# Turning K ahead of the exponentials' turns, and the normalised x one step later, in a fused attention and MLP kernel

## The chip, the cores and the metric

One core of one Trainium2 chip runs the whole program. The metric is the device time of one execution in microseconds. All stages are one launch; nothing is computed on the host but the layout of the arrays.

## The reference

`q`, `k`, `v` are (4 batches, 12 heads, 448 positions, 64). What matters here is the first part and what it hands on:

```python
def rmsnorm(x, g):
    rms = np.sqrt(np.mean(x * x, axis=-1, keepdims=True) + 1e-06)
    return x / rms * g
q_n, k_n = (rmsnorm(q, g_q), rmsnorm(k, g_k))
scores = scale * np.matmul(q_n, k_n.transpose(0, 1, 3, 2))
scores = scores - np.max(scores, axis=-1, keepdims=True)
attn = np.exp(scores)
attn = attn / (np.sum(attn, axis=-1, keepdims=True) + 1e-09)
out = np.matmul(attn, v)                    # then x = out as (4, 448, 768)
# layer 1
xn = (x - mu) / np.sqrt(var + 1e-06) * g_ln
x = x + np.maximum(xn @ w_ch1, 0.0) @ w_ch2
# layer 2
u = x + (x.transpose(0, 2, 1) @ U @ V).transpose(0, 2, 1)
out = u + np.maximum(u @ w_ch1, 0.0) @ w_ch2
```

## The kernel before

The work of each engine is written out by hand in one list of entries, `seq`, which every engine's program walks in the same order. Its first part is attention: entries ("step", n), n from 0 to 101. The 48 heads make 24 pairs, `t`; the 448 query positions make four tiles, `i`, of 112. So n = 4t + i, and I call the four steps of one t a period, and a step by its i. From step 96 on the products of the first MLP are mixed in, and from step 102 on there are only products. Engines run freely against each other and meet by semaphores alone, so an engine works through its own list in order, and stands still at the first entry whose semaphore has not come.

In step n TensorE does, in this order: `score(n)` (L696, six products of high and low parts of q and k), `value(n-2)` (L717, e turned times v), `turn_e(n-1, h)` for both heads (L704, four transposes of a 112 x 448 tile of exponentials each). In the step with i = 2 come `turn_k(t+1)` (L684, four transposes of the normalised K of the next pair) and `turn_values(t-1)` (L726) behind it; in the steps with i = 3 `turn_x("x", ...)` (L738, the pair's attention output turned for the residual), and, in 18 of the steps, `turn_x("n", ...)` (the same line, the layer-normalised x turned for the MLP). All turns except K's go into two PSUM banks, `sc_ps`, used in turn; a bank is free again when ScalarE or VectorE has copied it out. With e(n-1, 0) and e(n-1, 1) before it, any third turn of a step goes into the bank of e(n-1, 0), which ScalarE copies in `copy_e` (L869). The other one is VectorE's (L1045).

ScalarE's step: `keep_x` (L880) or `keep_norm` (L897) for a turn of the step before, `make_high` (L917, in steps 65 to 92 with i under 3: inputs of the MLP), `copy_e(n-1)` (L869), `exponential(n)` (L857, one for each head, with an accumulator read behind each), at i = 2 `k_high(t+1)` (L848), at i = 1 `keep_values(t-1)` (L865) and `q_high(t+1)` (L843), and `normalise` (L888, half of the layer norm of a tile) one step ahead of the tile's turn. GpSimd does the other half (L630), the roots (L560, L565, L588), K's scaling `norm_k` (L570), `sums` (L577) and Q's low part (L581). VectorE does maxima (L1034, L1040), copies of e, K's low part `k_low` (L1026), sums of squares (L1018), `natural` (L1057) and statistics.

The table `XN_AT` says in which step each normalised tile is turned: tiles of batch 0 at steps 32, 36, ... 52 (i = 0), of batch 1 at 56, 57, 60, 64, 68, 72, of batch 2 at 80, 84, ... 96 and 100. `XN_AT`'s steps also set the time of the two halves of `normalise`, of `keep_norm`, and of the DMA that stores the tile.

Of the kernel before, what the change touches and what calls it, by code (L numbers as in the profile page):

```python
# [29 lines left out]
def mixer_kernel(nc, qkv, q_t, g_qk2, g_ln, u_lr, v_lr, w1, w2, out_t):  # L30
# [142 lines left out]
    with ExitStack() as ctx:  # L173
# [124 lines left out]


        XN_AT = {}  # L300
        for b, (first, order, ats) in enumerate(((32, (0, 1, 2, 3, 4, 5), (0, 4, 8, 12, 16, 20)),
                                                 (56, (0, 3, 1, 2, 4, 5), (0, 1, 4, 8, 12, 16)),
                                                 (80, (0, 1, 2, 3, 4, 5), (0, 4, 8, 12, 16, 20)))):
            for c, at in zip(order, ats):
                XN_AT[first + at] = PB * b + c
        xn_no = {t: k for k, t in enumerate(list(XN_AT.values()) + list(range(NP_ - PB, NP_)))}

        def xn_pair(n):
            return XN_AT.get(n)
# [93 lines left out]
        with nc.Block() as block:  # L403
# [135 lines left out]
            def _(pool):  # L539
# [99 lines left out]
                for what, n in seq:  # L639
                    if what == "step":  # L640
                        t, i = divmod(n, NI)
                        if i == 0:
                            for s, c, k in sum_made_at.get((what, n), ()):
                                make_sum(s, c, k)
                            if xn_pair(n + 1) is not None:
                                normalise(xn_pair(n + 1))
                        if i == 0 and t + 1 < NP_:
                            root_k(t + 1)
                            norm_k(t + 1)
                            root_q(t + 1)  # L650
                        if i == 1 and 1 <= t <= NP_:
                            sums(t - 1)
                        if i == 2 and t + 1 < NP_:
                            q_low(t + 1)
                        if i == 3 and t + 2 < NP_:
                            squares(t + 2)
                        if i == 0 and t >= 1 and (t - 1) % PB == 0 and t > 1:
                            root_var((t - 1) // PB - 1)
                        if i == 3 and xn_pair(n + 1) is not None:
                            normalise(xn_pair(n + 1))  # L660
                        if i != 0:
                            for s, c, k in sum_made_at.get((what, n), ()):
                                make_sum(s, c, k)
                        continue
                    for r, k in sums_at.get(n, ()):
                        weight_sum(r, k)
                    if what == "prod":
                        for s, c, k in sum_made_at.get((what, n), ()):
                            make_sum(s, c, k)

            @block.tensor
            def _(pe):
# [6 lines left out]
                def turn_k(t):  # L679
                    pe.wait_ge(kn_done, t + 1)  # L680
                    wait(pe, av_done, t - 1)
                    to = k_turned(t)
                    for i in range(NI):
                        last = nc.tensor.transpose(to[:, i * TP:(i + 1) * TP], kn[:, i], ident[:TP, :TP])  # L684
                    last.then_inc(kt_done, 1)
# [126 lines left out]
                for what, n in seq:  # L812
                    if what == "step":
                        if n < N:
                            score(n)
                        if 1 <= n <= 2:
                            warm((7, 6)[n - 1])
                        if 0 <= n - 2 < N:
                            value(n - 2)
                        for h in range(2):  # L820
                            if 0 <= n - 1 < N:
                                turn_e(n - 1, h)
                        if n % NI == 2 and n // NI + 1 < NP_:
                            turn_k(n // NI + 1)
                        if n % NI == 2 and 1 <= n // NI <= NP_:
                            turn_values(n // NI - 1)
                        if xt_pair(n) is not None:
                            turn_x("x", xt_pair(n))
                        if xn_pair(n) is not None:
                            turn_x("n", xn_pair(n))  # L830
                    if what == "prod":
                        if ln3_pair(n - 2) is not None:
                            turn_x("n", ln3_pair(n - 2))
                        if (at := mix_of(n)):
                            mixing(*at)
                        product(n)

            @block.scalar
            def _(act):
# [119 lines left out]
                for what, n in seq:  # L959
                    if what == "step":  # L960
# [6 lines left out]
                            make_high(s, c, k)  # L967
                        if 0 <= n - 1 < N:
                            copy_e(n - 1)
                        if n < N:  # L970
                            exponential(n)
                        if i == 2 and t + 1 < NP_:
                            k_high(t + 1)
                        if i == 1 and 1 <= t <= NP_:
                            keep_values(t - 1)
                        if i == 1 and t + 1 < NP_:
                            q_high(t + 1)
                        if xn_pair(n + 1) is not None:
                            normalise(xn_pair(n + 1))
# [283 lines left out]
```

## Time and profile before

| | |
|---|---|
| median of 3 runs | 1703.59 us (1701.42 to 1703.87) |
| profiled execution | 1705.68 us, its span 1703.7 us |
| PE busy over the span | 1666.4 us (98%), weight loads 1486.2 us (87%) |
| DVE, ACT, POOL busy | 1097.4, 701.5, 484.2 us |
| the chain that ended last | PE 80%, of it the products L770 41% and L760 35% |
| attention, until the first product of the MLP | 349.66 us of the span |

In the views PE is TensorE, PEld its weight loads, DVE VectorE, ACT ScalarE, POOL GpSimd and SP the queue that issues the DMAs. Times are in us from the span's start. In a timeline a row says when the first instruction of a group started and how long the group lasted; brackets say how long the engine had been idle before it, and what released it. On ACT and PE a row's duration overlaps with the next row's start, since instructions are pipelined: the time that one takes in the queue is read from start to start.

### The profile page before, as it was taken

To read this page: it belongs to the slowest core of one execution; us is meant where nothing else is said; L and a number is where in the kernel's file an instruction comes from. 1 tells how busy PE (TensorE), PEld (TensorE's weight loads), DVE (VectorE), ACT (ScalarE), POOL (GpSimd) and SP (SyncE) were. 2 spreads that over 40 slices of the span, in tenths; PEclk is the share of its full clock that TensorE was granted. 3 is DMA by queue.
4 is the path that set the end of the run, shared out by engine and by line. 5 is a ranking of instruction groups with operands and counts; after the bars stand their busy time and mean duration, and the time that the engine had idled before them with its cause. 6 is when DMAs were issued, how large, how long until landed. Compare 5 with 4: busy or idle time off the path is not lost.

```text
span 1703.7 us, 27419 instructions
## 1 busy us (share of the span) xinstructions
PE 1666.4 (98%) x10040; PEld 1486.2 (87%) x10040; DVE 1097.4 (64%) x2072; ACT 701.5 (41%) x1648; POOL 484.2 (28%) x434
## 2 busy tenths in 40 slices
PE   9999988899999999999999999999999999999999
PEld 7767666689999999999999999999999999999998
DVE  6878788866555559665555496656555975555654
ACT  5777888752233224332232243223322432223321
POOL 5667778711111114211021132110111321111110
PEclk9999999999999999999999999999999999999999
DMA  4223334221112114422221145122211451111112
GB/s 122 76 73 88 93 104 132 65 91 65 67 67 75 42 59 158 169 78 77 78 78 61 55 164 183 62 75 81 93 49 67 164 171 44 62 62 56 56 56 84
DMA packets 54867, 149.29 MB, mean 88 GB/s; under 512 B 6000, under 2 KB 36848, under 8 KB 54736
## 3 DMA queue, kind: packets, MB, share of 16 engines
q1 hardware_dynamic: 54736, 147.55, 26.5%
q8 instruction: 82, 1.34, 0.3%
q14 instruction: 49, 0.40, 0.1%
HBM read 122.75 MB, written 24.77 MB: 87 GB/s over the span
## 4 chain that ended last, share of the span: by engine, by line
PE 80%; DVE 1%; ACT 1%; issue 1%; POOL 1%; DVEq 0%; ACTq 0%; POOLq 0%
PE mm_ps L770 41%; PE mm_ps L760 35%; PE sc_ps L782 1%; PE sc_ps L792 1%; PE mm_ps L717 0%; PE mm_ps L696 0%; PE sc_ps L738 0%; ACT e_nat L857 0%; PE sc_ps L800 0%; PE sc_ps L704 0%; DVE mm_ps L1034 0%; DVE h_lo L1100 0%; ACT e_t L869 0%; DVE qk_ss L1018 0%; POOL make L601 0%
## 5 line engine op out<-in xcount | busy, mean ns | idle before, releaser
L770 PE MATMUL mm_ps<-h_hi,w_hi 128*128 128x448 f32 x1152 | 423.1, 367 | 0.0
L770 PE MATMUL mm_ps<-h_hi,w_lo 128*128 128x448 f32 x1152 | 421.0, 365 | 0.0
L770 PE MATMUL mm_ps<-h_lo,w_hi 128*128 128x448 f32 x1152 | 420.9, 365 | 0.0
L1133 DVE TENSOR_TENSOR acc<-mm_ps,acc 128x448 f32<-128x448 f32 x288 | 166.2, 618 | 362.0 <-PE mm_ps L770 362.0
L760 PE MATMUL mm_ps<-in_hi,w_hi 128*128 128x448 f32 x1008 | 371.3, 368 | 0.0
L760 PE MATMUL mm_ps<-in_hi,w_lo 128*128 128x448 f32 x1008 | 368.3, 365 | 0.0
L760 PE MATMUL mm_ps<-in_lo,w_hi 128*128 128x448 f32 x1008 | 368.2, 365 | 0.0
L907 ACT ACTIVATE w_hi<-w_raw 128x256 fp32r<-128x256 f32 (+1 forms) x480 | 204.5, 452 | 188.7 <-PE mm_ps L770 168.1
L770 PEld LDWEIGHTS mm_ps<-h_hi,w_lo 128*128 128x128 f32 x1152 | 216.4, 188 | 17.6
L770 PEld LDWEIGHTS mm_ps<-h_lo,w_hi 128*128 128x128 f32 x1152 | 216.5, 188 | 17.0
L770 PEld LDWEIGHTS mm_ps<-h_hi,w_hi 128*128 128x128 f32 x1152 | 216.4, 188 | 17.0
L1087 DVE TENSOR_TENSOR w_lo<-w_raw,w_hi 128x256 fp32r<-128x256 f32 (+1 forms) x480 | 229.4, 491 | 0.3
L760 PEld LDWEIGHTS mm_ps<-in_hi,w_lo 128*128 128x128 f32 x1008 | 189.3, 188 | 15.3
L941 ACT ACTIVATE h_hi<-ht 128x448 fp32r<-128x448 f32 x144 | 83.4, 579 | 289.0 <-DVE ht L1118 155.7
L760 PEld LDWEIGHTS mm_ps<-in_lo,w_hi 128*128 128x128 f32 x1008 | 189.5, 188 | 14.6
L760 PEld LDWEIGHTS mm_ps<-in_hi,w_hi 128*128 128x128 f32 x1008 | 189.3, 188 | 14.6
L623 POOL TENSOR_TENSOR w_s<-w_raw,w_s 128x384 f32<-128x384 f32 x48 | 50.2, 1046 | 510.5 <-DVE w_lo L1087 510.5
L623 POOL TENSOR_TENSOR w_s<-w_raw 128x384 f32<-128x384 f32 x48 | 56.4, 1176 | 477.0 <-DMA w_raw<-in_w 407.7
L857 ACT ACTIVATE e_nat<-mm_ps,nbias,rs 112x448 f32<-112x448 f32 x192 | 137.5, 726 | 13.8 <-DVE nbias L1040 13.8
L1100 DVE SCALAR_TENSOR_TENSOR h_lo<-ht,h_hi 128x448 fp32r<-128x448 f32 x144 | 109.1, 758 | 32.2 <-ACT h_hi L941 32.1
L907 ACT ACTIVATE w_hi<-w_s 128x384 fp32r<-128x384 f32 x144 | 73.9, 517 | 116.2 <-POOL w_s L623 68.8
L1034 DVE TENSOR_REDUCE mm_ps<-mm_ps 112x2 f32<-112x896 f32 x96 | 104.8, 1092 | 9.1 <-PE mm_ps L696 9.0
(105 smaller groups left out, 1976.8 us busy)
## 6 DMA issues: line engine op xcount, KB each, us to landing
w_raw<-in_w SPq DMA_DIRECT2D x96, 768.0 KB, 4.3
qk<-in_qkv SPq DMA_DIRECT2D x23, 448.0 KB, 3.7
acc<-xres SPq DMA_DIRECT2D x6, 1344.0 KB, 9.8
qt_raw<-in_q_t SPq DMA_DIRECT2D x24, 224.0 KB, 2.6
v<-in_qkv SPq DMA_DIRECT2D x24, 224.0 KB, 2.7
xnrm<-st_n SPq DMA_DIRECT2D x24, 224.0 KB, 2.0
xres<-acc SPq DMA_DIRECT2D x24, 224.0 KB, 2.2
xa<-xres SPq DMA_DIRECT2D x24, 224.0 KB, 2.7
```

Of the source, the lines that this page charges most:

```text
L623: nc.gpsimd.tensor_tensor(out, in0, in1, op).then_inc(sum_done, 1)
L760: last = nc.tensor.matmul(bank(q), w[a][:, c * P:(c + 1) * P], x[:, k, c], start=k not in ONTO and c == 0 and p == 0, stop=c == HC - 1 and ...
L770: last = nc.tensor.matmul(bank(q, b), w[a][:, c * P:(c + 1) * P], x[:, half, 2 * c + b], start=half == 0 and c == 0 and p == 0, stop=half ...
L782: last = nc.tensor.matmul(sc_ps[1][:, :2 * P], u_st[:, i].rearrange("p n r -> p (n r)"), x[:], start=i == 0 and x is xs_hi, stop=i == NI - ...
L792: last = nc.tensor.transpose(sc_ps[0][:TP, e * P:(e + 1) * P], xa[:, e, i * TP:(i + 1) * TP], ident[:])
L857: nc.scalar.activation(e_nat[:, n % 3, h], mm_ps[:TP, 2 * (n % 2) + h, :S], ACT.Exp, bias=nbias[:, n % 2, h:h + 1], scale=rs[:, t % 2, 0, ...
L907: nc.scalar.activation(w_hi[:, q % RING, :width(q)], weights(q), ACT.Copy).then_inc(whi_done, 1)
L941: nc.scalar.activation(h_hi[:, g % 2, h], src, ACT.Relu).then_inc(hhi_done, 1)
L1034: nc.vector.reduce_max(nmax(n), mm_ps[:TP, 2 * (n % 2):2 * (n % 2) + 2, :S], axis=AX, negate=True).then_inc(max_done, 1)
L1087: nc.vector.tensor_tensor(w_lo[:, q % RING, :w], weights(q), w_hi[:, q % RING, :w].bitcast(F32), ALU.subtract).then_inc(wlo_done, 1)
L1100: nc.vector.scalar_tensor_tensor(h_lo[:, g % 2, h], src, 0.0, h_hi[:, g % 2, h].bitcast(F32), ALU.max, ALU.subtract).then_inc(hlo_done, 1)
L1133: nc.vector.tensor_tensor(acc[:, b, d], bank(q, b), acc[:, b, d], ALU.add).then_inc(ev_done, 1)
```

## The change

K's transposes stand ahead of e's on TensorE, K's high part ahead of the exponentials on ScalarE, Q's high part one step sooner, and the tiles in `XN_AT` are turned one step later (one of the last batch stays at step 100). GpSimd's half of `normalise` stays in the same step as before (it is called two steps ahead now), ScalarE's moves with the table.

```diff
-        for b, (first, order, ats) in enumerate(((32, (0, 1, 2, 3, 4, 5), (0, 4, 8, 12, 16, 20)),
-                                                 (56, (0, 3, 1, 2, 4, 5), (0, 1, 4, 8, 12, 16)),
-                                                 (80, (0, 1, 2, 3, 4, 5), (0, 4, 8, 12, 16, 20)))):
+        for b, (first, order, ats) in enumerate(((33, (0, 1, 2, 3, 4, 5), (0, 4, 8, 12, 16, 20)),
+                                                 (57, (0, 3, 1, 2, 4, 5), (0, 1, 4, 8, 12, 16)),
+                                                 (81, (0, 1, 2, 3, 4, 5), (0, 4, 8, 12, 16, 19)))):
...
-                            if xn_pair(n + 1) is not None:
-                                normalise(xn_pair(n + 1))
+                            if xn_pair(n + 2) is not None:
+                                normalise(xn_pair(n + 2))
...
-                        if i == 3 and xn_pair(n + 1) is not None:
-                            normalise(xn_pair(n + 1))
+                        if i == 3:
+                            for u in (xn_pair(n + 1), xn_pair(n + 2)):
+                                if u is not None:
+                                    normalise(u)
...
+                        if n % NI == 2 and n // NI + 1 < NP_:
+                            turn_k(n // NI + 1)
                         for h in range(2):
                             if 0 <= n - 1 < N:
                                 turn_e(n - 1, h)
-                        if n % NI == 2 and n // NI + 1 < NP_:
-                            turn_k(n // NI + 1)
...
+                        if i == 2 and t + 1 < NP_:
+                            k_high(t + 1)
                         if n < N:
                             exponential(n)
-                        if i == 2 and t + 1 < NP_:
-                            k_high(t + 1)
                         if i == 1 and 1 <= t <= NP_:
                             keep_values(t - 1)
-                        if i == 1 and t + 1 < NP_:
+                        if i == 0 and t + 1 < NP_:
                             q_high(t + 1)
```

On TensorE, in a step with i = 2 (here step 10, from its value product on: L717 value, L704 e's turns, L684 K's, L726 the values' turn, then the next score), before:

```order
L717 MATMUL mm_ps<-e_t,v 64x112 x8
L704 MATMUL sc_ps<-ident,e_nat 112x112 x8
L684 MATMUL mm_ps<-ident,qk_sq 128x112 x4
L726 MATMUL sc_ps<-ident,av 112x128 x4
L696 MATMUL mm_ps<-k_hi,q_hi 112x448 x2
```

and with the change, where lines stand two further down in the file:

```order
L719 MATMUL mm_ps<-e_t,v 64x112 x8
L686 MATMUL mm_ps<-ident,qk_sq 128x112 x4
L706 MATMUL sc_ps<-ident,e_nat 112x112 x8
L728 MATMUL sc_ps<-ident,av 112x128 x4
L698 MATMUL mm_ps<-k_hi,q_hi 112x448 x2
```

K's four transposes moved from between e's and the values' turns to ahead of e's, so that the values' turn follows e's directly.

On ScalarE, in steps 35 to 38, that is from the copy of e in step 35 (i = 3) to the one of step 38 (i = 2), before (L869 copy of e, L857 exponentials, L888 normalise, L880 keep x, L897 keep the normalised x, L865 keep values, L843 Q's high part, L848 K's):

```order
L869 ACTIVATE e_t<-sc_ps 112x448
L857 ACTIVATE e_nat,esum<-mm_ps,nbias,rs 112x448 x2
L888 ACTIVATE x_nat<-x_nat,shift,rstd 112x128 x2
L880 ACTIVATE acc<-sc_ps 128x448
L869 ACTIVATE e_t<-sc_ps 112x448
L857 ACTIVATE e_nat,esum<-mm_ps,nbias,rs 112x448 x2
L897 ACTIVATE st_n<-sc_ps,g_col 128x448
L869 ACTIVATE e_t<-sc_ps 112x448
L857 ACTIVATE e_nat,esum<-mm_ps,nbias,rs 112x448 x2
L865 ACTIVATE av<-mm_ps 128x448
L843 ACTIVATE q_hi<-qt_raw 128x448
L869 ACTIVATE e_t<-sc_ps 112x448
```

and with the change:

```order
L871 ACTIVATE e_t<-sc_ps 112x448
L859 ACTIVATE e_nat,esum<-mm_ps,nbias,rs 112x448 x2
L882 ACTIVATE acc<-sc_ps 128x448
L871 ACTIVATE e_t<-sc_ps 112x448
L859 ACTIVATE e_nat,esum<-mm_ps,nbias,rs 112x448 x2
L845 ACTIVATE q_hi<-qt_raw 128x448
L890 ACTIVATE x_nat<-x_nat,shift,rstd 112x128 x2
L871 ACTIVATE e_t<-sc_ps 112x448
L859 ACTIVATE e_nat,esum<-mm_ps,nbias,rs 112x448 x2
L867 ACTIVATE av<-mm_ps 128x448
L899 ACTIVATE st_n<-sc_ps,g_col 128x448
L871 ACTIVATE e_t<-sc_ps 112x448
```

Q's high part and both normalising instructions now stand between the exponentials of the step with i = 0 and the copy of e in the step with i = 1; the other steps have lost one or the other. The orders of GpSimd and VectorE are the same before and after; on SP only the stores of the normalised x stand one step later.

## Rows read from the trace of the kernel before

**Rows 1.** Windows: length, busy us of PE, PEld, DVE, ACT, POOL; granted clock; DMA.

```profile
62.15:75.14 12.99, 12.19 (x133) 9.16 (x132) 10.72 (x22) 9.69 (x26) 7.55 (x6) 1.00 0.25 72
143.53:156.94 13.41, 12.71 (x139) 9.51 (x138) 10.89 (x22) 10.86 (x29) 9.11 (x9) 1.00 0.29 87
302.14:316.16 14.02, 12.72 (x137) 9.53 (x137) 12.39 (x25) 12.29 (x32) 9.89 (x10) 1.00 0.22 67
...
0.00:349.66 349.66, 317.15 (x3293) 240.03 (x3293) 277.98 (x546) 265.95 (x652) 235.41 (x206) 0.99 0.31 92
349.66:1703.70 1354.04, 1349.26 (x6751) 1246.13 (x6749) 819.45 (x1527) 435.52 (x996) 248.78 (x228) 1.00 0.26 87
```

**Rows 2.** TensorE's waits in attention: waiter, releaser: us in total, times, longest.

```profile
PE sc_ps L738 <- ACT e_t L869: 10.1, 30, 0.3
PE mm_ps L717 <- DVE e_t L1045: 4.8, 11, 0.9
PE mm_ps L696 <- DVE k_lo L1026: 4.7, 6, 1.6
PE sc_ps L738 <- POOL x_nat L630: 4.4, 3, 2.2
PE sc_ps L726 <- ACT e_t L869: 4.3, 9, 0.5
...
PE sc_ps L704 <- ACT st_x L880: 0.8, 2, 0.6
```

**Rows 3.** Timeline of TensorE in step 18 (i = 2, a period without normalised x).

```profile
68.70 0.99 PE L717 MATMUL mm_ps<-e_t,v 112*64 112x112 f32 x16 [0.37 <-DVE e_t L1045]
69.62 0.98 PE L704 MATMUL sc_ps<-ident,e_nat 112*112 112x112 f32 x8
70.44 0.55 PE L684 MATMUL mm_ps<-ident,qk_sq 112*128 112x112 f32 x4
71.06 0.62 PE L726 MATMUL sc_ps<-ident,av 128*112 128x128 f32 x4
```

**Rows 4.** Timeline of GpSimd and ScalarE beside that step.

```profile
68.65 1.04 POOL L570 TENSOR_TENSOR qk_sq<-qk,rs 112x512 f32<-112x512 f32 x1
69.91 0.58 ACT L843 ACTIVATE q_hi<-qt_raw 128x448 fp32r<-128x448 f32 x1
70.37 0.55 ACT L869 ACTIVATE e_t<-sc_ps 112x448 f32<-112x448 f32 x1
```

**Rows 5.** Timeline of ScalarE, steps 39 and 40 (i = 3 and 0), with normalised x.

```profile
142.33 0.54 ACT L869 ACTIVATE e_t<-sc_ps 112x448 f32<-112x448 f32 x1 [1.10 <-PE sc_ps L704]
142.77 0.72 ACT L857 ACTIVATE e_nat<-mm_ps,nbias,rs 112x448 f32<-112x448 f32 x1
...
144.18 0.87 ACT L888 ACTIVATE x_nat<-x_nat,shift,rstd 112x128 f32<-112x128 f32 x2
144.95 0.54 ACT L880 ACTIVATE acc<-sc_ps 128x448 f32<-128x448 f32 x1
145.87 0.54 ACT L869 ACTIVATE e_t<-sc_ps 112x448 f32<-112x448 f32 x1 [0.39 <-PE sc_ps L704]
```

**Rows 6.** Timeline of TensorE in step 40: e's turns, then the normalised x's.

```profile
145.24 0.98 PE L704 MATMUL sc_ps<-ident,e_nat 112*112 112x112 f32 x8
146.56 0.57 PE L738 MATMUL sc_ps<-ident,x_nat 112*128 112x112 f32 x4 [0.34 <-ACT e_t L869]
```

**Rows 7.** Timeline of ScalarE and TensorE in step 86 (i = 2, with the MLP's inputs made).

```profile
310.91 0.58 ACT L917 ACTIVATE in_hi<-make 128x448 fp32r<-128x448 f32 x1
...
312.07 0.62 PE L726 MATMUL sc_ps<-ident,av 128*112 128x128 f32 x4 [0.54 <-ACT e_t L869]
```

**Rows 8.** Timeline of TensorE in steps 88 and 89: the longest wait, and what follows it.

```profile
321.02 0.86 PE L738 MATMUL sc_ps<-ident,x_nat 112*128 112x112 f32 x4 [2.17 <-POOL x_nat L630]
...
323.20 1.67 PE L717 MATMUL mm_ps<-e_t,v 112*64 112x112 f32 x16
```

**Rows 9.** Timeline of TensorE at step 32, the first of a period behind a late K.

```profile
115.52 0.46 PE L696 MATMUL mm_ps<-k_hi,q_hi 64*112 64x448 f32 x2 [0.93 <-DVE k_lo L1026]
```

## The prediction

> **What bounds the kernel now.** I first took the busy time of each engine by stage [rows 1]. From 349.66 us on TensorE is busy 1349.26 of 1354.04 us: nothing in the change touches that stage but its first steps, and whatever attention gains or loses shifts all of it. Before, TensorE is busy 317.15 of 349.66 us, so some 32 us of idleness are all that can be won. It is near to being the bound in every kind of period: 12.19 of 12.99 us in a plain one, 12.71 of 13.41 with a normalised x, 12.72 of 14.02 where the MLP's inputs are made too. ScalarE's share goes up from 9.69 to 10.86 and 12.29 us in the same three windows: in the last it has 1.7 us left in 14, so the place of a work in its queue matters more than its length. Then I read who TensorE waits for [rows 2]: the turns of x wait for ScalarE's copy of e 30 times, 0.34 us each, value for VectorE's copy 11 times, the values' turn for ScalarE's copy 9 times. Three waits for GpSimd make 4.4 us, six for K's low part 4.7. Last I read the timeline of a plain and of two fuller periods [rows 3 to 9].
>
> One relation carries the argument. A third turn of a step needs the bank that ScalarE empties: e's turns start at 145.24, the copy at 145.87 (0.63 later, when the first head is turned), the next turn at 146.56 (0.69 after the copy's start) [rows 5, 6]. So behind a turn of e, any third turn starts 1.32 us after e's start; e's eight transposes themselves take 0.82 (69.62 to 70.44) [rows 3].
>
> **K ahead of e's turns.** Nothing is added or removed, and K's high part isn't what the next score waits for: VectorE takes it up a step later. In a plain period K's transposes fill the time in which ScalarE copies: e's turn 69.62, K's 70.44, the values' 71.06 [rows 3], which is 0.69 after the copy's start at 70.37 [rows 4]. With K first, e's turn starts later by K's transposes: four instead of eight, so half of 0.82, 0.41 us. K is also ready only at 69.69 (68.65 and 1.04) [rows 4], against the slot at 69.62: some 0.1 more. That gives e's turn at 70.13, the copy at 70.76, the values' turn at 71.45: 0.4 us late. Bounds: 0.3, if GpSimd's end costs nothing and ScalarE, freed of Q's high part, copies with no delay; 0.5 with a later K. I take 0.4. Exponentials start later too, but they have over 1 us of slack: ScalarE idles 1.10 us ahead of the next copy [rows 5]. Steps 4 to 27 hold 6 such periods: **+2.4 us**. In the period that ends in step 31, VectorE gets its sums late from GpSimd and the next score waits 0.93 us for K's low part [rows 9]; the delay vanishes in that wait. I count the same for the other three periods that end in a large wait of this kind: 0.
>
> In periods with a normalised x but no MLP inputs, ScalarE was hardly late, so the same move costs K's 0.41 less a tenth by which the two copies of e had been late there: 0.3. Where inputs are made, ScalarE does them between Q's high part and the copy (310.91), and the values' turn waited up to 0.54 us [rows 2, 7]. Q's high part gone from there, and K first: I count 0.2 won.
>
> **Normalised x one step later, Q's high part sooner.** Take step 40 of before. ScalarE copies e at 145.87; 0.44 later the exponentials (as 142.33 to 142.77), which with their reads take 1.41 (142.77 to 144.18): it is free at 147.72. Q's high part costs 0.46 from start to start (69.91 to 70.37) and the two normalising instructions 0.77 (144.18 to 144.95) [rows 4, 5]. Before, the second stood at the end of step 39, where 0.39 us of idleness were still left behind keep x, the first a step later. Now both follow the exponentials: ScalarE is free at 148.95. Without x's turn, step 41's score starts at 145.24 + 0.82, say 146.1; e's turn comes 1.71 later (143.53, the window's start, to 145.24), with a little wait for VectorE at 147.9, and can be copied from 148.5 [rows 1, 5, 6]. The copy is 0.45 us late, and with it x's turn and all behind it. Together with K's 0.3: +0.75 for each of 4 periods (steps 36 to 51), **+3.0**. Bounds of this lateness: 0, if the high part of Q or the normalising slips into idle time, to 0.9. The period with two turns (57, 58) I put at +0.4, the one of 61 at +0.2, the last (no K, no Q) at +0.1.
>
> Where MLP inputs are made, one more instruction of some 0.48 from start to start (0.58 long) [rows 7] stands ahead of that copy: 0.93 late, less the 0.2 of K: +0.7. That holds in 4 periods (turns at 65, 73, 81, 85): **+2.8**. In the other two GpSimd was late, and a step's delay hides that. The three waits for it are 4.4 us, one of 2.17 and two of 1.1 [rows 2, 8]. For the turn at 69: 0.8 comes back of the 1.1, since 0.34 stays, against 0.7: 0. For the one at 81 I give nothing back, a choice: VectorE was late in that period as well, and puts the exponentials and the copy behind them back. For 89: x's turn waited 2.17 us, and TensorE then ran its value product in 1.67 us instead of 0.99 [rows 3, 8]; with e's turns (0.82) slowed in the same proportion that is 1.2 us for the fallen clock. 1.83 and 1.2 us come back, less 0.93, and K gives 0.2 but GpSimd's K is as much late: **-2.1**.
>
> Steps 32 to 35: the wait of 0.93 [rows 9] shrinks to some 0.5, since 0.4 of it now lies in step 30; if a fallen clock behind it (1.2 us) stays up instead, it is a gain of 0.5 beside the period's +0.7, and I put it at 0.1. At the end, normalise leaves the place ahead of keep x, where e's turn waited up to 0.6 us for the bank [rows 2]: **-0.6**. The stores of x move by a step of some 3.5 us and are needed 3 steps later: nothing.
>
> The Trainium skill (ScalarE: Activation LUTs, What ACT_TABLE_LOAD costs) says that back-to-back ACTIVATEs overlap by about 93 ns. The trace agrees: a copy lasts 0.54 us and holds the queue 0.44 [rows 5]. Costed by their durations, Q's part and the normalising would take 0.2 us more per period, and the sum would be some 2 us larger; I go by starts.
>
> **Sum.** 2.4 + 3.0 + 0.7 + 2.8 + 0 - 2.1 + 0.1 - 0.6 = +6.3 us. The profiled execution took 1705.68 us, so its like would take 1712.0; it was 2.1 us over the median of 1703.59, and against that I predict **1709.9 us**, 0.37% slower. What a measurement of this kernel can tell from no change is about 0.2%, 3.4 us.
>
> **Rivals.**
> *The queue on ScalarE isn't late (faster).* If the copy of e in steps with i = 1 comes on time, because the exponentials are through sooner than from 146.31 to 147.72 or the turn itself comes later, the terms for x shrink: 4 x 0.45 and 4 x 0.85 go, the two odd periods gain 0.9 each, the small ones 0.5: 7.5 us less, so -1.2. That decides from 0.4 us on in periods without MLP inputs and 0.9 us in those with them. A clock that then stays up behind the two longest waits for K's low part (up to 1.6 us [rows 2]), at 1.2 us each, brings it to -3.6: 1700.0, 0.2% faster. For it speaks that every one of the 4.4 us of waits for GpSimd goes; against it that ScalarE's queue is in order and its idleness ahead of the copy was 0.39 us in step 40 [rows 5], less than the 1.23 us that now come before.
> *The clock falls more often (slower still).* Behind the wait of 2.17 us the value product took 1.67 us [rows 8]. Full periods now have 0.34 + 0.93, near 1.3 us, of idleness in one place. Attention's granted clock is 0.99 as a whole [rows 1], so it fell seldom in before, with waits of 1.1 us among the rest; I don't count it. In four periods at 1.2 us each it is +4.8: 1714.7. The Trainium skill (TensorE: Matmul & The Clock Gate, Part 1) describes this: idleness halves the clock from 2.4 to 1.2 GHz and activity brings it back; the 1.67 us against 0.99 fit the lower level.
> *The waits only move (same).* If more of the K delay ends in a wait for K's low part or for VectorE's copy of e (0.37 in every plain period, 4.8 us in all [rows 2]), its 2.4 and the 1.2 in the next term vanish: +2.7, 1706.3. Against it: VectorE's copy comes ahead of K in the step, and its chain begins at the e turn of i = 0, which shifts along.
>
> **How the numbers follow.** Forecast, +4 to +9: 0.50. Clock: 0.13. Waits only move: 0.19. ScalarE not late: 0.18. The range reaches from the faster rival to beyond the clock's, since the bounds for ScalarE's lateness are wide: 1699.5 to 1716. Slower by over 0.2%: 0.63; within: 0.19; faster: 0.18.
>
> **What would show it.** Plain periods of 13.4 instead of 12.99 us, with the values' turn now waiting 0.3 to 0.4 us for ScalarE's copy in nearly every period, so that this wait grows from 4.3 to some 8 us. x's turns in steps with i = 1 waiting 0.7 to 1.3 us for the same copy: L738 on ACT up from 10.1 to some 17 us. The waits of L738 for GpSimd gone. If the first is wrong, K's transposes aren't 0.41; if the second is, ScalarE's queue was shorter than I counted. What follows 349.66 us should last as long as before, within 1 us.

## The result, and the profile after

| | before | changed |
|---|---|---|
| median of the runs side by side | 1702.63 us (5 runs, 1701.35 to 1703.87) | 1711.27 us (5 runs, 1710.62 to 1711.87) |
| ratio, 95% interval | | 1.0052, 1.0040 to 1.0063 |
| profiled execution, its span | 1705.68, 1703.7 us | 1710.62, 1708.7 us |
| attention, until the first product of the MLP | 349.66 us | 353.90 us |

The changed kernel is 8.6 us slower, 0.52%. I had said 1709.9 us, slower by 0.37%. The first windows are the whole of attention and all that follows, with the columns of [rows 1]; the other three are a plain period, one with a normalised x, and one that makes the MLP's inputs too.

```profile
0.00:353.90 353.90, 311.32 (x3289) 235.06 (x3289) 274.67 (x545) 265.87 (x649) 235.16 (x206) 1.00 0.31 91
353.90:1708.70 1354.80, 1349.99 (x6755) 1246.44 (x6753) 817.34 (x1527) 437.11 (x1000) 249.07 (x228) 1.00 0.26 86
...
63.93:77.71 13.78, 12.25 (x134) 9.18 (x133) 10.62 (x22) 9.79 (x26) 7.53 (x6) 1.00 0.23 68
147.66:161.78 14.12, 12.72 (x137) 9.53 (x136) 10.76 (x22) 10.92 (x29) 9.10 (x9) 1.00 0.28 83
309.17:323.76 14.59, 12.72 (x138) 9.54 (x137) 12.29 (x25) 12.36 (x32) 9.70 (x9) 1.00 0.20 64
```

Most of it lies in attention: 4.2 of the 5.0 us between the two profiles. The part behind it lasts 1354.80 us against 1354.04 [rows 1], and half of these 0.8 us is a border that moved: before, the normalised x of step 96 is turned at 349.31 us, just ahead of the first product; with the change, at step 97, it is turned at 356.84, behind it, and takes 0.37 us there. The busy times of each kind of period are those of before, and only the lengths have grown: 13.78 for 12.99, 14.12 for 13.41, 14.59 for 14.02. So work was not added; TensorE stands still for longer. Whom it waits for in attention, with the columns of [rows 2]:

```profile
PE sc_ps L740 <- ACT e_t L871: 21.3, 38, 1.2
PE sc_ps L728 <- ACT e_t L871: 7.7, 23, 0.3
PE mm_ps L719 <- DVE e_t L1047: 4.8, 10, 0.9
PE mm_ps L686 <- ACT av L867: 4.2, 9, 0.5
PE mm_ps L698 <- DVE k_lo L1028: 2.2, 4, 0.9
```

Against [rows 2], x's turns wait 21.3 us for ScalarE's copy of e instead of 10.1, the values' turn 7.7 instead of 4.3. The 4.4 us of waits for GpSimd's half of the normalising are gone, and K's low part costs 2.2 instead of 4.7. The fourth row has no counterpart in [rows 2]: **K's turn (L686) waits for ScalarE's copy of the kept values (L867)**, nine times, 0.47 us in the typical case. My prediction doesn't mention it. The step-18 timeline of TensorE, ScalarE and GpSimd, the place of [rows 3, 4], shows where it comes in:

```profile
70.44 1.04 POOL L570 TENSOR_TENSOR qk_sq<-qk,rs 112x512 f32<-112x512 f32 x1
...
70.49 0.99 PE L719 MATMUL mm_ps<-e_t,v 112*64 112x112 f32 x16 [0.37 <-DVE e_t L1047]
...
71.27 0.54 ACT L867 ACTIVATE av<-mm_ps 128x448 f32<-128x448 f32 x1
...
71.94 0.57 PE L686 MATMUL mm_ps<-ident,qk_sq 112*128 112x112 f32 x4 [0.47 <-ACT av L867]
72.36 0.93 PE L706 MATMUL sc_ps<-ident,e_nat 112*112 112x112 f32 x8
72.94 0.54 ACT L871 ACTIVATE e_t<-sc_ps 112x448 f32<-112x448 f32 x1 [1.14 <-PE sc_ps L706]
...
73.63 0.62 PE L728 MATMUL sc_ps<-ident,av 128*112 128x128 f32 x4 [0.34 <-ACT e_t L871]
```

GpSimd has K ready at 71.48 (70.44 and 1.04), and TensorE's value product is through at about the same time. But K is turned into the bank `mm_ps[:, 4 + t % 2]`, in which the values of the pair two before it (same remainder of t) were summed up, so `turn_k` has a second wait, on `av_done`: ScalarE must have copied those values out. That copy stands behind the exponentials of the step with i = 1 and ends at 71.81. K starts at 71.94. Before, the same copy stood here in step 18, beside [rows 4]:

```profile
69.48 0.54 ACT L865 ACTIVATE av<-mm_ps 128x448 f32<-128x448 f32 x1
```

It ended at 70.02, 0.4 us behind the slot at 69.62 into which K was to move. But e's eight transposes stood in that slot, K came at 70.44, and the wait was covered; K's position was what paid for it.

**Two profiles of the same kernel.** The difference of the two profiled spans is 5.0 us, that of the medians 8.6. So I profiled before once more (run e8_before_again below). Here are its windows, and TensorE at the place of [rows 8], from it:

```profile
0.00:345.78 345.78, 312.84 (x3292) 236.41 (x3293) 278.13 (x546) 266.17 (x652) 236.10 (x206) 1.00 0.32 93
345.78:1699.60 1353.82, 1349.02 (x6751) 1246.17 (x6749) 818.28 (x1527) 435.82 (x996) 249.45 (x228) 1.00 0.26 87
...
318.65 0.60 PE L738 MATMUL sc_ps<-ident,x_nat 112*128 112x112 f32 x4 [2.16 <-POOL x_nat L630]
...
319.97 0.99 PE L717 MATMUL mm_ps<-e_t,v 112*64 112x112 f32 x16
```

The wait of 2.16 us is there as in [rows 8], but the value product behind it lasts 0.99 us, not 1.67. The granted clock (the column ahead of the last two) behind this wait, TensorE alone, first in the first profile and then in the second:

```profile
322.00:324.00 2.00, 2.00 (x14) 0.50 0.29 108
318.65:322.00 3.35, 3.35 (x36) 1.00 0.21 72
```

Attention is 345.78 us long instead of 349.66, with a granted clock of 1.00 instead of 0.99. The first profile of before holds 3.9 us that this one doesn't: three places at which TensorE fell to the lower of its two levels (1.2 instead of 2.4 GHz) behind a wait, 1.2 us each, at steps 32, 64 and 88, and 0.3 us of smaller shifts. Against the second profile the change costs 1708.7 - 1699.6 = 9.1 us, near the 8.6 of the medians. In what follows I compare with the second one where a clock fall would blur a number.

By period (step n = 4t), the change against both profiles of before, in us, with what I had predicted:

| part | predicted | first profile | second profile |
|---|---|---|---|
| up to step 4 | 0 | -0.6 | -0.5 |
| six plain periods, t = 1 to 6 | +2.4 | +4.7 | +4.7 |
| t = 7, 13, 19 (end in a wait for K's low part) | 0 | -0.3 | -0.3 |
| t = 8 (begins with step 32) | +0.1 | -0.5 | +0.7 |
| four with a normalised x, t = 9 to 12 | +3.0 | +2.9 | +2.9 |
| t = 14 and 15 (steps 56 to 63) | +0.6 | +0.1 | +0.1 |
| t = 16, 18, 20, 21 (MLP inputs) | +2.8 | +1.4 | +2.5 |
| t = 17 (turn at 69) | 0 | -0.1 | -0.1 |
| t = 22 (turn at 89) | -2.1 | -2.2 | -0.6 |
| step 92 to the first product | -0.5 | -1.2 | -1.2 |
| behind it | 0 | +0.8 | +1.0 |
| sum | +6.3 | +5.0 | +9.1 |

Rounded as they are, the rows of the last column add up to 9.2. Some 0.4 us of the last two parts is the turn of x that changed sides.

### The profile page after: what moved, and what is told of

Its sections match the earlier page's. It is cut to its first block, busy times and chain, and to the rows that moved or that the text cites. A ratio compares the mean times of both kernels' runs of the same rounds, so it can differ in the third digit from the quotient of the medians.

```text
span 1708.7 us, 27419 instructions
## 1 busy us (share of the span) xinstructions
PE 1661.3 (97%) x10040; PEld 1481.5 (87%) x10040; DVE 1092.0 (64%) x2072; ACT 703.0 (41%) x1648; POOL 484.2 (28%) x434
## 4 chain that ended last, share of the span: by engine, by line
PE 80%; DVE 1%; ACT 1%; issue 0%; DVEq 0%; ACTq 0%
PE mm_ps L772 41%; PE mm_ps L762 35%; PE sc_ps L784 1%; PE mm_ps L719 1%; PE sc_ps L794 1%; PE mm_ps L698 1%; PE sc_ps L706 0%; PE sc_ps L740 0%; ACT e_t L871 0%; PE sc_ps L802 0%; ACT e_nat L859 0%; DVE mm_ps L1036 0%; DVE h_lo L1102 0%; PE sc_ps L728 0%; DVE x_nat L1015 0%
## 5 line engine op out<-in xcount | busy, mean ns | idle before, releaser
L762 PEld LDWEIGHTS mm_ps<-in_hi,w_hi 128*128 128x128 f32 x1008 | 189.4, 188 | 14.4
```

The source lines that it names most:

```text
L762: last = nc.tensor.matmul(bank(q), w[a][:, c * P:(c + 1) * P], x[:, k, c], start=k not in ONTO and c == 0 and p == 0, stop=c == HC - 1 and ...
```

## The experiments

Two theories stood. The first (A): K in front of e's turns costs nearly all of it, since its turn waits for the copy of the kept values, and with it 0.8 us in every plain period. The second, my prediction's: K costs 0.4 where nothing covers it, and the queue of ScalarE with the later normalised x and Q's high part costs the larger half, 3.5 of 6.3 us or more. In the texts on record and below, "before" is the kernel before, run beside each experiment, whose median was between 1702.4 and 1703.1 us.

### One part alone

**e1_k_alone**: before, with nothing but K moved, on TensorE and on ScalarE.

```diff
+                        if n % NI == 2 and n // NI + 1 < NP_:
+                            turn_k(n // NI + 1)
                         for h in range(2):
                             if 0 <= n - 1 < N:
                                 turn_e(n - 1, h)
-                        if n % NI == 2 and n // NI + 1 < NP_:
-                            turn_k(n // NI + 1)
...
+                        if i == 2 and t + 1 < NP_:
+                            k_high(t + 1)
                         if n < N:
                             exponential(n)
-                        if i == 2 and t + 1 < NP_:
-                            k_high(t + 1)
```

> Only K's part of the change: K's turn ahead of e's on TensorE, K's high part ahead of the exponentials. Theory A (the wait for the bank that the kept values leave is what K's turn pays for, and it is paid in every period whose i = 2 step isn't followed by a larger wait): in plain periods i = 2 steps last 4.9 instead of 4.14 us, and since Q's high part and the kept values still stand right ahead of the copy, the step grows by some 0.8 us in the periods with a normalised x too and by 0.4 where MLP inputs are made; TensorE waits for L865's copy in more than 15 steps; total +9 to +12 us against before, more than the whole change. Rival B (K first costs only its own transposes, 0.3 to 0.4 us a period, and the normalised x costs the rest): +4 to +6 us.

Measured: 1711.75 us, ratio 1.0053 (1.0039 to 1.0066), +9.3 us. K alone costs as much as the whole change. TensorE's waits in attention:

```profile
PE sc_ps L738 <- ACT e_t L869: 11.6, 35, 0.3
PE sc_ps L726 <- ACT e_t L869: 7.9, 23, 0.3
PE mm_ps L684 <- ACT av L865: 7.5, 17, 0.5
```

x's turns wait as before, the values' turn as in the changed kernel, and K's turn waits 17 times for the kept values, 7.5 us in all. Here the periods with a normalised x have the wait too: +0.78 in each of t = 9 to 12. K's high part ahead of the exponentials was not tried apart from K's turn; but TensorE's matmuls wait for no exponential, here or in the changed kernel, so nothing speaks for a cost of its own.

**e2_x_and_q**: the changed kernel with both moves of K taken back, so that the later normalised x and the sooner Q remain.

```diff
-                        if n % NI == 2 and n // NI + 1 < NP_:
-                            turn_k(n // NI + 1)
                         for h in range(2):
                             if 0 <= n - 1 < N:
                                 turn_e(n - 1, h)
+                        if n % NI == 2 and n // NI + 1 < NP_:
+                            turn_k(n // NI + 1)
...
-                        if i == 2 and t + 1 < NP_:
-                            k_high(t + 1)
                         if n < N:
                             exponential(n)
+                        if i == 2 and t + 1 < NP_:
+                            k_high(t + 1)
```

> The other part alone: normalised x one step later and Q's high part sooner, K where it was. Theory A: steps with i = 1 and a normalised x last 4.0 us (4.45 with MLP inputs) as in the changed kernel, steps with i = 2 shrink to 3.6 us, since nothing is ahead of the copy of e; the waits for GpSimd go. Total -3 to +1 us against before. Rival B (the later x is the costly part): +3 to +5 us.

Measured: 1702.41 us (11 runs; one of them took 5706.63 us and is not in the ratio), ratio 0.9998 (0.9989 to 1.0007). These two parts cost nothing together, where I had counted half of the loss. Yet the late copy that I had worked out is there, in this kernel as in the changed one:

```profile
PE sc_ps L740 <- ACT e_t L871: 19.4, 36, 1.3
...
PE mm_ps L698 <- DVE k_lo L1028: 3.9, 6, 1.2
...
PE sc_ps L706 <- DVE stats L1069: 1.3, 2, 0.7
```

Against the second profile of before, a plain period gains 0.12 (ScalarE's copy in the step with i = 2 is no longer late behind Q's high part), a period with a normalised x loses 0.31, the one with the wait of 2.16 us gains 1.5 and the end some 1.2.

The two parts are not additive by period. In t = 9 to 12 K alone costs 0.78 and x with Q 0.31, together 0.72. The steps with i = 1 are longer there in the changed kernel (3.99 us at step 37, before 2.62), so that ScalarE has copied the values before TensorE comes to K: one delay covers the other. In plain periods nothing covers it, and K on top of x and Q costs 0.90. Where MLP inputs are made (t = 18 and 21), K alone costs 0.3, x with Q 0.2, together 0.6.

### Taking the wait away

**e3_values_first**: the changed kernel, with the copy of the kept values in front of the exponentials in the step with i = 1.

```diff
-                        if n < N:
-                            exponential(n)
                         if i == 1 and 1 <= t <= NP_:
                             keep_values(t - 1)
+                        if n < N:
+                            exponential(n)
```

> The changed kernel with the values kept ahead of the exponentials of the step with i = 1 on ScalarE instead of behind them. Theory A: K's turn no longer waits 0.47 us for that copy in plain periods, but for GpSimd's K some 0.1 us; steps with i = 2 fall from 4.93 to 4.5 us in 7 to 9 periods, total 2.5 to 3.5 us below the changed kernel (about 1708). If K's turn was held by K's scaling on GpSimd anyway: no change, 1711.

Measured: 1708.17 us (1708.05 to 1708.51), 3.1 us below the changed kernel, ratio to before 1.0032 (1.0019 to 1.0045). The same step 18:

```profile
68.30 0.54 ACT L867 ACTIVATE av<-mm_ps 128x448 f32<-128x448 f32 x1
...
69.37 0.99 PE L719 MATMUL mm_ps<-e_t,v 112*64 112x112 f32 x16 [0.37 <-DVE e_t L1047]
...
70.42 0.60 PE L686 MATMUL mm_ps<-ident,qk_sq 112*128 112x112 f32 x4
70.86 0.93 PE L706 MATMUL sc_ps<-ident,e_nat 112*112 112x112 f32 x8
...
72.13 0.62 PE L728 MATMUL sc_ps<-ident,av 128*112 128x128 f32 x4 [0.34 <-ACT e_t L871]
```

The values are out at 68.84 and no longer hold K's turn. It starts 1.05 us behind the value product's start, where e's turn started 0.92 behind it before [rows 3]: GpSimd has K ready only at 70.36, the 0.1 that I had counted. A plain period now costs 0.40 over before, which is the term that I had predicted: without the bank's wait, my step was right. The other periods are as in the changed kernel.

**e7_k_values_first**: the same move in e1_k_alone.

```diff
+                        if i == 1 and 1 <= t <= NP_:
+                            keep_values(t - 1)
                         if n < N:
                             exponential(n)
-                        if i == 1 and 1 <= t <= NP_:
-                            keep_values(t - 1)
```

> K's part alone (as the run k alone), with the values kept ahead of the exponentials on ScalarE. Theory A: the 0.39 to 0.47 us of waiting for the kept values go in 17 steps, the rest of K first stays: i = 2 steps 4.5 us in plain periods, 4.1 with a normalised x; 5 to 7 us below K alone (1711.75): about 1706. Rival (the wait is really for GpSimd's K): 1709 to 1711.

Measured: 1707.80 us, 4.0 below e1_k_alone, ratio 1.0026 (1.0017 to 1.0034); each against the before beside it, +4.7 instead of +9.3. A plain period costs 0.40, one with a normalised x 0.35. My expectation was 5 to 7, a miss: K then meets its other feeder in the fuller periods (8 waits for GpSimd's scaling, 2.8 us). So 4.6 of the 9.3 us of K are the wait for the bank, 4.0 of them in the periods t = 1 to 6 and 9 to 12; of the 4.7 left, K's transposes in front of the copy make 3.8 in these ten periods (six by 0.40 and four by 0.35).

### The late copy on ScalarE

**e4_norm_early**: the changed kernel, with ScalarE's half of the normalising back in the step with i = 3 for the turns that come two steps later.

```diff
-                        if xn_pair(n + 1) is not None:
-                            normalise(xn_pair(n + 1))
+                        for u in (xn_pair(n + 1) if i == 3 else None, xn_pair(n + 2) if i in (3, 0) else None):
+                            if u is not None:
+                                normalise(u)
```

> The changed kernel with ScalarE's half of the normalising back in the step before (i = 3), as it was for a turn at i = 0, while x is still turned at i = 1. Theory A: the copy of e in i = 1 is on time again; x's turn waits 0.34 us instead of 0.71 and 1.17; the step lasts 3.62 instead of 3.99 and 4.45 us in 12 periods, total 6 to 8 us below the changed kernel (about 1704.5). If the normalising wasn't what made the copy late (Q's high part alone): under 2 us less.

Measured: 1709.11 us (1708.53 to 1710.09), ratio 1.0038 (1.0025 to 1.0050): only 2.2 us below the changed kernel, a miss. The changed kernel at step 41 first, with ScalarE's queue from the copy of step 40 on:

```profile
150.01 0.54 ACT L871 ACTIVATE e_t<-sc_ps 112x448 f32<-112x448 f32 x1 [1.16 <-PE sc_ps L706]
...
151.85 0.58 ACT L845 ACTIVATE q_hi<-qt_raw 128x448 fp32r<-128x448 f32 x1
152.08 0.98 PE L706 MATMUL sc_ps<-ident,e_nat 112*112 112x112 f32 x8
152.32 0.87 ACT L890 ACTIVATE x_nat<-x_nat,shift,rstd 112x128 f32<-112x128 f32 x2
...
153.09 0.53 ACT L871 ACTIVATE e_t<-sc_ps 112x448 f32<-112x448 f32 x1
...
153.77 0.57 PE L740 MATMUL sc_ps<-ident,x_nat 112*128 112x112 f32 x4 [0.71 <-ACT e_t L871]
```

and the same step in e4:

```profile
151.96 0.98 PE L706 MATMUL sc_ps<-ident,e_nat 112*112 112x112 f32 x8
...
152.59 0.54 ACT L871 ACTIVATE e_t<-sc_ps 112x448 f32<-112x448 f32 x1 [0.28 <-PE sc_ps L706]
153.27 0.57 PE L740 MATMUL sc_ps<-ident,x_nat 112*128 112x112 f32 x4 [0.34 <-ACT e_t L871]
```

The copy starts 0.63 after the turn instead of 1.01, x's turn waits 0.34 instead of 0.71, and all of L740's waits for ScalarE fall from 21.3 to 13.6 us: the edit did what it was made for. But periods of t = 9 to 12 win 0.34 each and three of the four with MLP inputs only some 0.3 (t = 16: 0.67) of the 0.76 to 0.90 that their step with i = 1 became shorter. With that step shorter, K's turn comes before the copy of the values again, and waits 0.46 (K on `av`: 6.4 us in all, from 4.2), value waits 0.86 for VectorE's copy of e in step 90, and at the end e's turn waits for the bank of x as it did before (0.8 us again). The cover of the last section, taken away, gives the price back.

**e6_all_fixed**: e4 and e3 together (its diff is those two).

> The whole change, with ScalarE's normalising in the step before and the values kept ahead of the exponentials. Theory A: what is left of K first is its own transposes and GpSimd's end, 0.3 to 0.4 us a period; K's turn waits no more for the kept values. i = 2 steps 4.5 us in plain periods, 4.0 with a normalised x. 4 to 5 us below the run with the normalising alone put back (1709.1): about 1704.5, and still 5 to 7 us above the same kernel with K where it was. Rival: K's wait for the kept values is replaced by a wait for K's scaling on GpSimd, over 1707.

Measured: 1707.35 us, ratio 1.0020 (1.0011 to 1.0029). I had expected about 1704.5, and the rival came (over 1707): the wait for the kept values is gone, that of x's turns is as in e4, and K's turn waits for its other feeder, GpSimd:

```profile
PE sc_ps L740 <- ACT e_t L871: 13.1, 36, 0.6
...
PE mm_ps L686 <- POOL qk_sq L570: 2.9, 8, 0.9
```

A plain period still costs 0.42 us, one with a normalised x 0.34, one with MLP inputs 0.2 to 0.3 over before (t = 18, 20 and 21; t = 16 nothing). That is what K's place costs when ScalarE holds up neither K nor x.

### Without K's move

**e5_no_k_norm_early**: e2 with the normalising as in e4.

> K where it was, normalised x turned one step later, Q's high part sooner, and ScalarE's half of the normalising in the step before (i = 3). Theory A (the two costs are separate: K's turn in front, and ScalarE's late copy of e in i = 1): both are absent, only the gains are left (waits for GpSimd gone, the values' turn not behind Q's high part): steps with i = 1 and a normalised x 3.6 us, with i = 2 3.6 us; 3 to 6 us below before, 1696.5 to 1699.5. If ScalarE's lateness only moves on to the i = 2 step: 1701 to 1703.

Measured: 1701.32 us, ratio 0.9985 (0.9976 to 0.9994), 1.8 us below before and 6.0 below e6, which differs from it in K's place and the values' copy. I had expected 1696.5 to 1699.5; it is the other case, that the lateness moves on to the step with i = 2. In the periods with MLP inputs the time went on to the next step: there e's second turn waits for the bank of the normalised x (L899, `keep_norm`), 3.0 us in six waits, since ScalarE's queue has exponentials and the values' copy in front of it. In step 86:

```profile
306.17 0.72 ACT L859 ACTIVATE e_nat<-mm_ps,nbias,rs 112x448 f32<-112x448 f32 x1 [0.78 <-DVE nbias L1043]
...
307.59 0.54 ACT L867 ACTIVATE av<-mm_ps 128x448 f32<-128x448 f32 x1
...
308.01 0.64 ACT L899 ACTIVATE st_n<-sc_ps,g_col 128x448 f32<-128x448 f32 x1
...
308.80 0.57 PE L706 MATMUL sc_ps<-ident,e_nat 112*112 112x112 f32 x4 [0.46 <-ACT st_n L899]
```

ScalarE idles 0.78 us for VectorE's maxima ahead of those exponentials, so the values' copy fits in there for nothing.

**e9_no_k_values_first**: e5 with the values' copy in front of the exponentials, the edit of e3.

> The kernel of the run no k, norm early (1701.3), with the values kept ahead of the exponentials in i = 1. There TensorE's second turn of e waits 0.37 to 0.46 us for ScalarE's copy of the normalised x (L899) in five i = 2 steps, 0.87 in one, while ScalarE idles 0.78 us ahead of the exponentials of the step before. If the copy of the values fits into that idleness (0.42 us from start to start), those waits go: 2 to 3 us less, about 1699. If VectorE's maxima end before it is through: 0 to 1 us less.

Measured: 1700.67 us (11 runs, 1698.85 to 1703.52), ratio 0.9986 (0.9977 to 0.9995). The waits for L899 fell from 3.0 us to 0.4. The median hardly moved, though (1701.32 before it, and the ratios to before are the same), where I had expected 2 to 3 us less. The runs with a granted clock of 1.0 took 1698.85 to 1699.24 us, against 1700.43 and 1700.49 in e5; before's own at 1.0 were some 0.4 us lower beside e9, so about 1 us was won there. The others took up to 1703.5, and waits for K's low part grew from 4.3 to 5.7 us. What was won in one wait is in part idleness of another.

**e10_root_later**: e9, with the roots of the layer norm (`root_var`, GpSimd, once for each batch) behind the sums of the next step.

```diff
                         if i == 1 and 1 <= t <= NP_:
                             sums(t - 1)
+                        if i == 1 and t >= 1 and (t - 1) % PB == 0 and t > 1:
+                            root_var((t - 1) // PB - 1)
...
-                        if i == 0 and t >= 1 and (t - 1) % PB == 0 and t > 1:
-                            root_var((t - 1) // PB - 1)
```

> The same, and GpSimd's root of the variance one step later, behind the sums of the exponentials (L577). At three places (steps 31, 55, 79) the sums now wait for it, and K's low part and the next score behind them, 0.65 to 0.94 us at the score and 0.6 to 0.75 at e's turn. If that root is what is late: some 1 us less at each, 2 to 4 us below the run before, about 1696. If VectorE would be as late without it: within 1 us of it.

Measured: 1696.90 us (1696.63 to 1697.74), ratio 0.9964 (0.9951 to 0.9976): 6.0 us faster than before, 14.4 faster than the changed kernel. GpSimd's sums in the period that ends in step 31 start at 109.40 instead of 110.96 us. TensorE in steps 31 and 32, first in e9:

```profile
112.72 0.57 PE L706 MATMUL sc_ps<-ident,e_nat 112*112 112x112 f32 x4 [0.58 <-DVE stats L1070]
113.12 0.55 PE L740 MATMUL sc_ps<-ident,x_nat 112*128 112x112 f32 x4
114.60 0.46 PE L698 MATMUL mm_ps<-k_hi,q_hi 64*112 64x448 f32 x2 [0.93 <-DVE k_lo L1029]
```

and in e10:

```profile
111.24 0.98 PE L706 MATMUL sc_ps<-ident,e_nat 112*112 112x112 f32 x8
112.56 0.58 PE L740 MATMUL sc_ps<-ident,x_nat 112*128 112x112 f32 x4 [0.34 <-ACT e_t L871]
113.06 0.46 PE L698 MATMUL mm_ps<-k_hi,q_hi 64*112 64x448 f32 x2
```

Both waits are gone, step 31 takes 3.54 us instead of 4.77, and steps 55 and 79 are 0.76 and 0.95 shorter.

### The same kernels again

**e8_before_again** and **e11_after_again** are before and the changed kernel, unchanged, for a second profile each.

> The kernel before, unchanged, for a second profile. The first one's execution took 2.1 us more than the median and had TensorE's clock fall behind three waits (steps 32, 64 and 88, about 1.2 us each). If the falls are a matter of the execution, this one shows another number of them and a span that differs by some 1.2 us for each; if they belong to the kernel, the same three and a span of 1703.7.

> The changed kernel once more, for a second profile: its waits ahead of steps 32, 64 and 89 are 0.3, 0.9 and 1.2 us instead of 0.9, 1.6 and 2.2. If TensorE's clock falls behind long waits alone, it stays up here too: span 1708.7 to 1710, granted clock 1.0. If not, falls of 1.2 us each appear at other places.

Measured: before 1701.56 us, its span 1699.6, as shown above; the changed kernel 1711.17, its span 1709.3, its periods within 0.02 us of the first profile's, the part behind attention 0.6 us longer. The 27 runs of before beside e5 to e8 lie between 1701.6 and 1706.2 us and go by their granted clock: 1701.6 to 1702.0 at 1.0, 1702.7 to 1704.4 at 0.999 and 0.998, 1704.6 to 1706.2 below. The six runs of the changed kernel were all at 1.0.

## Why the prediction was right, and where it was not

Right: slower, both delays of the likeliest case are there, and the time is within the range: 1709.9 against 1711.27 us. The sum was +6.3 against +8.6 of the medians, 2.3 us short. That the times are only 1.4 us apart is luck: the median that I counted from was 1703.59, and the one beside the changed kernel 1702.63. It is luck too that the sum came so near, as the shares of K and of x in it were wrong.

**K in plain periods was the term mis-sized: 0.4 predicted, 0.78 measured, 2.3 us over six periods.** The step that fell short is "K is also ready only at 69.69 (68.65 and 1.04) [rows 4], against the slot at 69.62: some 0.1 more". I had asked when K's input is there, and not whether its output's place is free. In step 18 K starts 1.45 us behind the value product's start, where e's turn started 0.92 behind it (0.53 more, of it 0.47 of waiting for the kept values); K's transposes take 0.42; and from e's start to the values' turn it is 1.27 us instead of 1.44, since Q's high part no longer stands ahead of ScalarE's copy: 0.53 + 0.42 - 0.17 = 0.78 [rows 3, 4]. Shown by e1 (the wait, 17 times), and by e3, in which the wait is gone and the period costs 0.40. That the values' turn would wait 0.3 to 0.4 us nearly always, 8 us in all, came true (7.7), as did plain periods longer than 12.99, though at 13.78 and not 13.4. For that case I had written that K's transposes then aren't 0.41; they are 0.42, and the sign would have pointed past the bank.

**x and Q: the lateness of ScalarE's queue was right, its price in the total not.** I had x's turns wait some 17 us for the copy of e, and they wait 21.3; in step 41 the wait beyond the usual 0.34 is 0.37, where I had 0.45, and in steps with MLP inputs 0.83, where I had 0.93. The four periods gave +2.9 for +3.0, the four with MLP inputs +2.5 for +2.8. But by parts I had the shares wrong: e2 shows that x and Q together cost nothing (0.9998), since they also bring back 4.4 us of waits for GpSimd and the wait at the end, and shorten plain periods by 0.12 each. In t = 9 to 12 I had 0.30 for K and 0.45 for x; they are 0.41 and 0.31, and only because x's own delay covers the wait for the kept values there. Where MLP inputs are made I had K winning 0.2 and x losing 0.93; K on top of x and Q costs 0.4, and x with Q 0.2 (e2, t = 18 and 21).

**The waits for GpSimd went as forecast, and the clock did not.** I gave step 89 a gain of 2.1 us, 1.2 of it for the fallen clock behind the wait of 2.17 us. Against the first profile it is 2.2, against the second 0.6: the clock's part exists only in executions in which the clock falls. I had made the sum against one execution, with its falls, and carried it to the median by a shift of 2.1 us. But that shift stands for falls that the median run has fewer of; where the clock doesn't fall in before, the change can't win by keeping it up, so I counted that gain once too often. Against the second profile the terms of t = 22 and t = 8 are 2.1 us too low together, nearly as much as K's.

**Small terms.** The wait for K's low part at step 32 fell from 0.93 to 0.26 (I said 0.5), the end gave 1.2 instead of 0.5 (0.35 of it the turn of x that now lies behind the first product), t = 14 and 15 +0.1 instead of +0.6, the start half a microsecond and the products about one the other way. Of the rivals, none came: ScalarE is late, the clock did not fall more often, and waits did move to other places only in part.

The 0.5 us at the start come from no instruction that was moved. K's first turn stands behind TensorE's warm-up products (L807, L809 with the change), and the first 44 of them, the same in both, last longer in one kernel than in the other; first before, then changed:

```profile
1.56 7.85 PE L807 MATMUL mm_ps<-ident 128*128 128x128 f32 x44 [1.56 <-POOL ident L543]
1.56 6.71 PE L809 MATMUL mm_ps<-ident 128*128 128x128 f32 x44 [1.56 <-POOL ident L543]
```

From 3 to 6 us before has 16 matmuls and the changed kernel 22; before runs 6 or 7 in a microsecond up to 7 us and 10 or 11 from then on, the changed kernel 12 from 5 us on. Each kernel's second profile shows the same (7.78 and 6.55 us). The early rise is also in e3, e5, e6 and e10, the late one in e1, e2 and e4, and e7 and e9 lie between; that goes with none of the parts, and why it differs stays open.

What else stays open is the rest of the 0.8 to 1.0 us by which the part behind attention is longer. It goes with the later x: over the first profile of before it is 0.7 to 1.4 us in every kernel that has it, and -0.4 and 0.0 in e1 and e7, which don't. Of that 0.4 is the turn of x; the rest was not traced, and the two profiles of the changed kernel differ by 0.6 there.

## What to carry to other kernels

For an instruction that is moved forward, list every semaphore that it waits on and when each of them came in the trace before, those of the place it writes as well as those of what it reads: in the trace before, K's input was 0.07 us late for the new place, its bank 0.4 us. A place in the order that seems to cost nothing may be what hides a wait, and a delay may cover another, so the costs of parts measured alone (+9.3 and 0 us here) need not add up in each period. And before the sum is made against one profile, compare its granted clock with that of other executions: here 0.99 against 1.00 in attention was 3.9 us, nearly half the effect to be forecast.

## What the runs showed of the hardware

The same waits of TensorE led to a fall of the clock in one execution and not in another. Behind 0.93, 1.58 and 2.17 us of idleness (steps 32, 64 and 88) the first profile of before ran at the lower level for a while, at 1.2 us each, and the second, behind 0.93, 1.57 and 2.16 us at the same places, at full speed. The Trainium skill (TensorE: Matmul & The Clock Gate, Part 1) has idleness halve the clock; the rows agree that it happens behind idleness, but by these two executions the length of a wait alone doesn't decide it. Nor do the kernels settle it. In the changed kernel no wait is over 1.3 us once the steps run, and all six runs were at 1.0; but in e2 none is over 1.3 us either, and nine of its ten counted runs were at 0.997 to 0.999. In e10, whose longest wait is 1.6 us, all five were at 0.998 or 0.999. What decides it was not tested.
